# A dynamic convolution and a two-layer MLP: the leftover 64 rows of the first layer as two matmuls on halves of the array, chunks taken in groups of four

## The chip, the cores and the metric

The kernel runs on one core of a Trainium2 chip. The metric is the device time of one execution in microseconds (us); less is better. The profile and the trace come from one further execution, recorded by the hardware profiler.

## The reference

`x` is 4 x 4096 tokens of 192 features, `weight_gen` gives 8 heads x 7 taps for each token, and the MLP has weights of 192 x 2048 and 2048 x 192, all fp32. Cut to what matters:

```python
w = exp(weight_gen - max(weight_gen)); w = w / (sum(w) + 1e-09)      # over the 7 taps
out[b, s, h] = sum_k w[b, s, h, k] * x_pad[b, s + k, h]              # 8 heads of 24 features
h = out.reshape(16384, 192) @ w_in                                   # 2048 hidden features
return maximum(0.01 * h, h) @ w_out
```

## The kernel before, in words

**Precision.** Each fp32 operand of a matmul is scaled by a power of two and split into two fp16 numbers, a high part and a low part (the rest). A product is then the sum of high x high, high x low and low x high.

**Tiles.** The 16384 tokens make 32 tiles (`TILES`) of 512 (`NT`: 4 tokens in each of 128 partitions). The 2048 hidden features make 16 chunks of 128 (`NF`); `f` counts the chunks of a tile, `m` the tiles.

**TensorE** (PE, lines 591 to 706). For each chunk, `hidden` (L605) makes the first layer in five matmuls of 512 columns into one of two PSUM banks `h_ps`. The 192 input features are more than the 128 rows of the array. The first 128 take `whA` and `wlA` against the high part of x (L608, L609) and `whA` against its low part (L612). The other 64 are laid out so that high and low parts of x alternate in the 128 rows, and meet `whD` (L610) and `wlD` (L611), whose rows hold each of the 64 weight rows twice. `project` (L635) makes the second layer, for each of the four groups `j` of 128 tokens: one matmul of 384 columns with the high part `gh` as stationary operand against both parts of `w_out` (L626), and one of 192 columns with `gl` against the high part (L631). The sums lie in four banks of `out_ps`, the products with the high and with the low part of `w_out` side by side. The first layer runs three chunks ahead (`LAG`) of the second. In slot 11 of 16 come twelve transposes of the next tile's x (L599, L602).

**ScalarE** (ACT, L274). For each chunk, `leaky` reads `h_ps` twice: `gh` in fp16 (L304) and `g` in fp32 (L306). Once a tile it makes the high part of x (L295), copies the transposed x out of PSUM (L300), and in `copy_out` (L309) moves the half of `out_ps` that holds the products with the low part of `w_out` to `stage` (L317). Every second tile it takes the exponentials of the taps (L284).

**VectorE** (DVE, L368) makes the convolution of the coming tiles (`convolve`, L420: products L433, sums L440, then scales), the softmax of the taps, the low part of x (L464), one in four of the low parts `gl = g - gh` (L473), and in `sum_out` (L476) adds the two halves of the output (L480). **GpSimd** (POOL, L215) makes the other three of four `gl` (L227). Rings of four chunks hold `gh`, `gl` and `g`.

**Order.** Everything is placed by hand in 16 slots a tile: `CONV_IN_SLOT`, `SOFTMAX_IN_SLOT`, `X_HI_SLOT`, `X_LO_SLOT`, `TRANSPOSE_SLOT`. In tile 0 the weights are split in pieces as well, each of four chunks: the high part by ScalarE (L279, `HI_IN_SLOT`), then the low part by VectorE (L459, `LO_IN_SLOT`); TensorE waits for the pieces in `step` (L661). The **SP** queue (L235) loads x and taps a chunk of two tiles at a time, and stores each tile (`store`, L259).

## Time and profile before

| what | value |
|---|---|
| median of 3 runs | 1132.56 us (1132.48 to 1132.85) |
| profiled execution: its time | 1132.38 us |
| its span, first to last instruction | 1130.6 us |
| mean granted TensorE clock | 0.994 of full speed |
| busy: PE, PE weight loads, DVE, ACT, POOL | 96%, 57%, 74%, 61%, 51% of the span |
| moved by DMA | 43.02 MB, 38 GB/s on the mean |

How to read it: the span leaves out what lies around the instructions (1132.38 - 1130.6 = 1.8 us). Busy shares are means over the whole span, and matmuls overlap each other in the pipeline, so the distance from the start of one to the start of the next (the pitch) tells what one costs, not its own duration.

### The profile page before, as it was taken

How to read it: one execution, taken by the hardware profiler on the slowest of the kernel's cores; microseconds unless marked ns; L12 is line 12 of the kernel's file. 1: busy time of each engine (PE TensorE's matmuls, PEld its weight loads, DVE VectorE, ACT ScalarE, POOL GpSimd, SP SyncE). 2: the span in 40 equal slices, each digit the busy share in tenths (PEclk: the TensorE clock that was granted, in tenths of full speed). 3: DMA queues.
4: the chain of work that ended last, by engine and by line, in shares of the span. 5: the costliest groups of instructions: out<-in, count | busy, mean ns of one | idle time of the engine just before them, and what ended most of it. 6: DMA issues, size and time to landing. Idle time of an engine off the chain costs nothing.

```text
span 1130.6 us, 17224 instructions
## 1 busy us (share of the span) xinstructions
PE 1091.0 (96%) x7064; PEld 646.3 (57%) x7064; DVE 837.8 (74%) x1126; ACT 694.5 (61%) x1348; POOL 574.8 (51%) x392
## 2 busy tenths in 40 slices
PE   2689999999999999999999999999999999999998
PEld 0346565665555565556556555656555556556564
DVE  7877877768687677877768787777878767787730
ACT  3556666656666666656666666666666666666664
POOL 0245555555555545455555555555555555555533
PEclk9889999999999999999999999999999999999999
DMA  7010010101001010100101001010200101000000
GB/s 243 1 58 14 18 70 15 71 1 72 14 15 72 15 58 15 53 34 15 72 5 67 15 15 72 14 72 1 72 14 15 72 14 58 15 15 15 15 15 14
DMA packets 12102, 43.02 MB, mean 38 GB/s; under 512 B 1276, under 2 KB 5372, under 8 KB 9848
## 3 DMA queue, kind: packets, MB, share of 16 engines
q1 hardware_dynamic: 11900, 41.64, 10.0%
q8 instruction: 55, 0.90, 0.4%
q10 hardware_dynamic: 124, 0.29, 0.2%
q14 instruction: 23, 0.19, 0.1%
HBM read 29.34 MB, written 12.58 MB: 37 GB/s over the span
## 4 chain that ended last, share of the span: by engine, by line
PE 93%; DVE 5%; ACT 1%; DMA 0%; issue 0%; ACTq 0%; POOL 0%; DVEq 0%; POOLq 0%
PE out_ps L626 29%; PE out_ps L631 15%; PE h_ps L608 10%; PE h_ps L609 10%; PE h_ps L610 10%; PE h_ps L612 10%; PE h_ps L611 10%; PE t_ps L599 1%; DVE conv L440 1%; DVE prod L433 1%; PE t_ps L602 1%; DMA xbuf<-in_x_dram 0%; DVE wo L459 0%; ACT xs L295 0%; DVE xs L464 0%; DVE conv L433 0%
## 5 line engine op out<-in xcount | busy, mean ns | idle before, releaser
L227 POOL TENSOR_TENSOR gl<-g,gh 128x512 f16<-128x512 f32 x384 | 572.8, 1495 | 548.7 <-ACT g L306 548.6
L304 ACT ACTIVATE gh<-h_ps 128x512 f16<-128x512 f32 x512 | 304.9, 596 | 389.2 <-PE h_ps L612 385.2
L626 PE MATMUL out_ps<-wo,gh 128*128 128x384 f16 x2048 | 423.4, 327 | 0.0
L306 ACT ACTIVATE g<-h_ps 128x512 f32<-128x512 f32 x512 | 302.9, 592 | 0.0
L626 PEld LDWEIGHTS out_ps<-wo,gh 128*128 128x128 f16 x2048 | 198.7, 98 | 168.7 <-issue 1.9
L433 DVE TENSOR_TENSOR prod<-xbuf,taps 128x768 f32<-128x768 f32 x192 | 274.1, 1440 | 0.0
L631 PE MATMUL out_ps<-wo,gl 128*128 128x192 f16 x2048 | 258.6, 246 | 0.6 <-DVE gl L473 0.6
L473 DVE TENSOR_TENSOR gl<-g,gh 128x512 f16<-128x512 f32 x128 | 105.2, 822 | 180.4 <-ACT g L306 180.4
L631 PEld LDWEIGHTS out_ps<-wo,gl 128*128 128x128 f16 x2048 | 186.1, 98 | 71.7 <-DVE gl L473 1.0
L440 DVE TENSOR_TENSOR conv<-conv,prod 128x768 f32<-128x768 f32 x192 | 209.2, 1089 | 0.6
L608 PE MATMUL h_ps<-xT,whA 128*128 128x512 f16 x512 | 194.8, 380 | 7.3 <-DVE wo L459 3.8
L612 PE MATMUL h_ps<-xT,whA 128*128 128x512 f16 x512 | 194.8, 380 | 0.0
L609 PE MATMUL h_ps<-xT,wlA 128*128 128x512 f16 x512 | 194.8, 380 | 0.0
L610 PE MATMUL h_ps<-xT,whD 128*128 128x512 f16 x512 | 194.8, 380 | 0.0
L611 PE MATMUL h_ps<-xT,wlD 128*128 128x512 f16 x512 | 194.8, 380 | 0.0
L611 PEld LDWEIGHTS h_ps<-xT,wlD 128*128 128x128 f16 x512 | 50.3, 98 | 60.9 <-issue 0.8
L610 PEld LDWEIGHTS h_ps<-xT,whD 128*128 128x128 f16 x512 | 50.3, 98 | 60.9 <-issue 0.8
L612 PEld LDWEIGHTS h_ps<-xT,whA 128*128 128x128 f16 x512 | 50.2, 98 | 60.9 <-issue 0.8
L480 DVE SCALAR_TENSOR_TENSOR stage<-out_ps,out_scale,stage 128x192 f32<-128x192 f32 x128 | 44.6, 411 | 52.2 <-ACT stage L317 52.2
L608 PEld LDWEIGHTS h_ps<-xT,whA 128*128 128x128 f16 x512 | 50.2, 98 | 12.7 <-DVE wo L459 4.0
L317 ACT ACTIVATE stage<-out_ps,out_scale 128x192 f32<-128x192 f32 x128 | 43.4, 422 | 16.8 <-PE out_ps L631 16.8
L609 PEld LDWEIGHTS h_ps<-xT,wlA 128*128 128x128 f16 x512 | 50.2, 98 | 4.2 <-issue 0.3
(54 smaller groups left out, 428.3 us busy)
## 6 DMA issues: line engine op xcount, KB each, us to landing
xbuf<-in_x_dram SPq DMA_DIRECT2D x15, 1344.0 KB, 5.6
out_dram<-stage SPq DMA_DIRECT2D x32, 384.0 KB, 2.3
taps<-in_weight_gen_dram SPq DMA_DIRECT2D x16, 224.0 KB, 5.8
rawO<-in_moe_w_out_dram SPq DMA_DIRECT2D x4, 384.0 KB, 9.9
rawA<-in_moe_w_in_dram SPq DMA_DIRECT2D x1, 1024.0 KB, 7.5
rawD<-in_moe_w_in_dram SPq DMA_DIRECT2D x2, 512.0 KB, 8.7
xbuf<-in_x_dram SPq DMA_DIRECT2D x2, 384.0 KB, 5.7
xbuf<-in_x_dram SPq DMA_DIRECT2D x2, 72.0 KB, 4.2
```

Source lines behind the costliest of these rows:

```text
L227: nc.gpsimd.tensor_tensor(gl[:, f % G_RING, :], g[:, f % G_RING, :], gh[:, f % G_RING, :], ALU.subtract).then_inc(s_gl_p, 1)
L304: nc.scalar.activation(gh[:, f % G_RING, :], h_ps[f % 2][:], ACT.Prelu, scale=SHRINK, alpha=SLOPE).then_inc(s_gh, 1)
L306: nc.scalar.activation(g[:, f % G_RING, :], h_ps[f % 2][:], ACT.Prelu, scale=SHRINK, alpha=SLOPE).then_inc(s_g, 1)
L433: ins = nc.vector.tensor_tensor(dst.rearrange("p (r g) -> p r g", g=G), rows, w.to_broadcast([P, SUB * H, G]), ALU.mult)
L440: ins = nc.vector.tensor_tensor(acc, acc, prod[:, k % PRODS, :], ALU.add)
L608: nc.tensor.matmul(dst, whA[:, c], xT[:, par, 0, :], start=True, stop=False)
L609: nc.tensor.matmul(dst, wlA[:, c], xT[:, par, 0, :], start=False, stop=False)
L610: nc.tensor.matmul(dst, whD[:, c], xT[:, par, 1, :], start=False, stop=False)
L611: nc.tensor.matmul(dst, wlD[:, c], xT[:, par, 1, :], start=False, stop=False)
L612: nc.tensor.matmul(dst, whA[:, c], xT[:, par, 2, :], start=False, stop=True).then_inc(s_h, 1)
L626: nc.tensor.matmul(out_ps[:, j, 0:2 * D], gh[:, f % G_RING, j * P:(j + 1) * P], wo[:, f, :, :], start=f == 0, stop=False)
L631: ins = nc.tensor.matmul(out_ps[:, j, 0:D], gl[:, f % G_RING, j * P:(j + 1) * P], wo[:, f, 0, :], start=False, stop=f == NF - 1)
```

## The change

**First layer.** In place of five matmuls of 512 columns over 128 rows, a chunk has four of those and one of 512 columns over 64 rows. x is transposed in three blocks: its first 128 features (high), then features 128 to 191 (high) with features 0 to 63 (low), then features 64 to 191 (low). `whA` and `wlA` meet the first block, `whX` the second, `whC` the third. What is left, the low part of the last 64 weight rows against the high part of the last 64 features of x, is a matmul over 64 rows. For an even chunk it takes rows 0 to 63 of the array, for an odd chunk rows 64 to 127, from copies of `wlX` and of the transposed x (`xT_again`) that DMAs put there. The product of the two low parts of these 64 features, which `wlD` brought with it, is not made any more.

**Groups.** `hidden` and `project` work on groups of four chunks: sixteen full matmuls into four banks `h_ps`, then the four 64-row ones; then the second layer of the group before. The first layer is one group ahead. The rings hold eight chunks.

**Second layer.** The products with both parts of `w_out` are summed in the same 192 columns: two matmuls of 192 columns in place of one of 384. `out_ps` has two banks, each with the sums of two groups of tokens. `sum_out` is gone: ScalarE copies the finished sums to `stage`.

**Order.** Slots are replaced by four steps a tile; 9 of the 18 operations of a convolution run a tile ahead (5 before). VectorE makes `gl` of the last chunk of each group. The SP queue has `move_weights` (three DMAs for each of four pieces) and `move_x` (one DMA a tile), and a store is issued one tile later in its program.

The diff, cut to its core (lines that rename `whD`, `rawD` and the rings are left out):

```diff
-LAG = 3
-G_RING = 4
+GROUP = 4
+RING = 2 * GROUP
 PRODS = 3
 SLOPE = 0.01
-LO_PERIOD = 4
...
+CONV_AHEAD_IN = {2: 4, 3: 5}
+CONV_AHEAD = sum(CONV_AHEAD_IN.values())
+CONV_IN = {0: 4, 1: N_CONV - CONV_AHEAD - 4}
 
 N_SOFTMAX = 6
-SOFTMAX_IN_SLOT = {2: (0,), 3: (1,), 6: (2, 3), 7: (4,), 8: (5,)}
-EXP_SLOT = 4
+SOFTMAX_IN = {0: (0, 1), 1: (2, 3, 4, 5)}
...
+        xT_again = sb("xT_again", [P, 2, NT], F16)
...
-        gh = sb("gh", [P, G_RING, NT], F16)
-        gl = sb("gl", [P, G_RING, NT], F16)
-        g = sb("g", [P, G_RING, NT])
-
-        h_ps = [ps(f"h_ps{b}", [P, NT]) for b in range(2)]
+        gh = sb("gh", [P, RING, NT], F16)
+        gl = sb("gl", [P, RING, NT], F16)
+        g = sb("g", [P, RING, NT])
+
+        h_ps = [ps(f"h_ps{b}", [P, NT]) for b in range(GROUP)]
         t_ps = ps("t_ps", [P, 2, NT], F16)
         t2_ps = ps("t2_ps", [P, 2, NT], F16)
-        out_ps = ps("out_ps", [P, SUB, 512])
+        out_ps = ps("out_ps", [P, 2, 512])
...
+        HI_IN = [3, 3, 1, 0]
...
+        LO_IN = [3, 3, 1, 0]
...
+            return f % GROUP == GROUP - 1
+
+        def out_of(j):
+            return out_ps[:, j // 2, j % 2 * D:(j % 2 + 1) * D]
...
-            for half in range(2):
-
-                sp.dma_start(rawD[half:P:2, :], w_in[P:D, :]).then_inc(s_rawD, DMA)
+
+            sp.dma_start(rawX[0:DR, :], w_in[P:D, :]).then_inc(s_rawX, DMA)
+            sp.dma_start(rawX[DR:P, :], w_in[0:DR, :]).then_inc(s_rawX, DMA)
...
+            def move_weights(n):
+
+                c = slice(n * PIECE, (n + 1) * PIECE)
+                sp.wait_ge(s_w_hi, hi_done(("X", n)))
+                sp.dma_start(whC[0:DR, c], whA[DR:P, c]).then_inc(s_w_moved[n], DMA)
+                sp.dma_start(whC[DR:P, c], whX[0:DR, c]).then_inc(s_w_moved[n], DMA)
+                sp.wait_ge(s_w_lo, LO_ORDER.index(("X", n)) + 1)
+                sp.dma_start(wlX[DR:P, c], wlX[0:DR, c]).then_inc(s_w_moved[n], DMA)
+
+            def move_x(t):
+
+                sp.wait_ge(s_xT_a, t + 1)
+                sp.dma_start(xT_again[DR:P, t % 2, :], xT[0:DR, t % 2, 1, :]).then_inc(s_xT_again, DMA)
...
+            move_weights(0)
+            move_x(0)
+            for n in range(1, N_PIECES):
+                move_weights(n)
             for m in range(TILES):
+                if m > 0:
+                    store(m - 1)
                 if m % 2 == 0 and m // 2 + 2 < CHUNKS:
 
                     c = m // 2
                     sp.wait_ge(s_conv, (c * 2 + 2) * N_CONV)
                     load_chunk(c + 2, c % 2)
-                store(m)
+                if m + 1 < TILES:
+                    move_x(m + 1)
+            store(TILES - 1)
...
+            def leaky(n):
+
+                for f in range(n % NG * GROUP, (n % NG + 1) * GROUP):
+                    act.wait_ge(s_h, n // NG * NF + f + 1)
+                    nc.scalar.activation(gh[:, f % RING, :], h_ps[f % GROUP][:], ACT.Prelu, scale=SHRINK, alpha=SLOPE
+                                         ).then_inc(s_gh, 1)
+                    nc.scalar.activation(g[:, f % RING, :], h_ps[f % GROUP][:], ACT.Prelu, scale=SHRINK, alpha=SLOPE
+                                         ).then_inc(s_g, 1)
...
-                    nc.scalar.activation(stage[:, u, j, :], out_ps[:, j, D:2 * D], ACT.Copy,
-                                         scale=out_scale[:, u, j:j + 1]).then_inc(s_out_part, 1)
-
-            def step(m):
+                    nc.scalar.activation(stage[:, u, j, :], out_of(j), ACT.Copy, scale=out_scale[:, u, j:j + 1]
+                                         ).then_inc(s_out_free, 1)
+
+            def step(n):
+
+                m, i = n // NG, n % NG
                 last = m == TILES - 1
...
+                if i == 0 and m > 0:
+                    copy_out(m - 1)
+                if i == 0 and m % 2 == 0 and m + 2 < TILES:
+                    exp_taps(m // 2 + 1)
+                if i == 1 and not last:
+                    hi_of_x(m + 1)
+                if m == 0:
+                    for piece in HI_ORDER[HI_FIRST + sum(HI_IN[:i]):HI_FIRST + sum(HI_IN[:i + 1])]:
+                        split_hi(piece)
+                if i == 2 and not last:
+                    take_transposed(m + 1)
+                if n + 1 < NG * TILES:
+                    leaky(n + 1)
...
+                        if t >= 2:
+
+                            dve.wait_ge(s_out_free, SUB * (t - 1))
...
-                    nc.vector.scalar_tensor_tensor(xs[:, j, :, 1], conv[:, j, :], x_scale[:, j:j + 1], xs[:, j, :, 0],
+                    nc.vector.scalar_tensor_tensor(xs[:, j, D:2 * D], conv[:, j, :], x_scale[:, j:j + 1], xs[:, j, 0:D],
...
-            def sum_out(m):
-                u = m % 2
-                for j in range(SUB):
-                    dve.wait_ge(s_out_part, SUB * m + j + 1)
-                    nc.vector.scalar_tensor_tensor(stage[:, u, j, :], out_ps[:, j, 0:D],
-                                                   out_scale[:, u, j:j + 1], stage[:, u, j, :],
-                                                   ALU.mult, ALU.add).then_inc(s_out_free, 1)
...
+                if m % 2 == 0 and m + 2 < TILES:
+                    c = m // 2 + 1
+                    for k in SOFTMAX_IN.get(i, ())[0:2]:
+                        if k == 0:
+
+                            dve.wait_ge(s_chunk[c % 2], DMA * (c + 1))
+                        softmax(c, k)
+                if i in CONV_IN and not last:
+                    for k in range(CONV_IN[i]):
+                        convolve(m + 1, CONV_AHEAD + sum(CONV_IN[b] for b in range(i)) + k)
+                if i in CONV_AHEAD_IN and m + 2 < TILES:
+                    if i == 2 and m % 2 == 0:
+
+                        dve.wait_ge(s_softmax, N_SOFTMAX * (m // 2 + 1))
+                    for k in range(CONV_AHEAD_IN[i]):
+                        if k == 1:
+                            lo_of_g(n * GROUP + GROUP - 1, n % NG * GROUP + GROUP - 1)
+                        convolve(m + 2, sum(CONV_AHEAD_IN[b] for b in range(2, i)) + k)
+                else:
+                    lo_of_g(n * GROUP + GROUP - 1, n % NG * GROUP + GROUP - 1)
+                if m % 2 == 0 and m + 2 < TILES:
+                    for k in SOFTMAX_IN.get(i, ())[2:]:
+                        softmax(m // 2 + 1, k)
+                if m == 0:
+                    for piece in LO_ORDER[LO_FIRST + sum(LO_IN[:i]):LO_FIRST + sum(LO_IN[:i + 1])]:
+                        split_lo(piece)
+                if i == 1 and not last:
+                    lo_of_x(m + 1)
+                if i == 2 and not last:
+                    take_transposed(m + 1)
...
+            def hidden(n):
+                m, i = n // NG, n % NG
+                par = m % 2
+                fs = range(i * GROUP, (i + 1) * GROUP)
+                if i == 0:
+                    pe.wait_ge(s_xT_a, m + 1)
+                    pe.wait_ge(s_xT_v, m + 1)
+                for f in fs:
+                    c = slice(f * P, (f + 1) * P)
+                    dst = h_ps[f % GROUP][:]
+                    if n > 0:
+
+                        pe.wait_ge(s_g, m * NF + f - GROUP + 1)
+                    nc.tensor.matmul(dst, whA[:, c], xT[:, par, 0, :], start=True, stop=False)
+                    nc.tensor.matmul(dst, wlA[:, c], xT[:, par, 0, :], start=False, stop=False)
+                    nc.tensor.matmul(dst, whX[:, c], xT[:, par, 1, :], start=False, stop=False)
+                    nc.tensor.matmul(dst, whC[:, c], xT[:, par, 2, :], start=False, stop=False)
+
+                if i == 0:
+                    pe.wait_ge(s_xT_again, DMA * (m + 1))
+                for f in fs:
+                    c = slice(f * P, (f + 1) * P)
+                    if f % 2 == 0:
+                        ins = nc.tensor.matmul(h_ps[f % GROUP][:], wlX[0:DR, c], xT[0:DR, par, 1, :],
+                                               start=False, stop=True)
+                    else:
+                        ins = nc.tensor.matmul(h_ps[f % GROUP][:], wlX[DR:P, c], xT_again[DR:P, par, :],
+                                               start=False, stop=True)
+                    ins.then_inc(s_h, 1)
...
+                    pe.wait_ge(s_gl_v, (m * NF + f) // GROUP + 1)
...
+                    pe.wait_ge(s_gl_p, (m * NF + f) // GROUP * (GROUP - 1) + f % GROUP + 1)
...
+            def project(n):
+                m, i = n // NG, n % NG
+                fs = range(i * GROUP, (i + 1) * GROUP)
+                for f in fs:
+                    pe.wait_ge(s_gh, m * NF + f + 1)
+                    for j in range(SUB):
+                        if f == 0 and m > 0 and j % 2 == 0:
+
+                            pe.wait_ge(s_out_free, SUB * (m - 1) + j + 2)
+                        for part in range(2):
+                            nc.tensor.matmul(out_of(j), gh[:, f % RING, j * P:(j + 1) * P], wo[:, f, part, :],
+                                             start=f == 0 and j % 2 == 0 and part == 0, stop=False,
+                                             skip_group_check=True)
+                for f in fs:
                     wait_lo(m, f)
-                    project_lo(f, range(SUB))
-                elif f == NF - 1:
-                    project_hi(f, (0, 1))
-                    wait_lo(m, f)
-                    project_lo(f, (0, 1)).then_inc(s_out_ps, 1)
-                    project_hi(f, (2, 3))
-                    project_lo(f, (2, 3)).then_inc(s_out_ps, 1)
-                else:
-                    project_hi(f, range(SUB))
-                    wait_lo(m, f)
-                    project_lo(f, range(SUB))
+                    for j in range(SUB):
+                        ins = nc.tensor.matmul(out_of(j), gl[:, f % RING, j * P:(j + 1) * P], wo[:, f, 0, :],
+                                               start=False, stop=f == NF - 1, skip_group_check=True)
+                        if f == NF - 1 and j % 2 == 1:
+                            ins.then_inc(s_out_ps, 1)
...
+            def wait_w_in(n):
+
+                wait_piece(("A", n))
+                wait_piece(("X", n))
+                pe.wait_ge(s_w_moved[n], 3 * DMA)
+
+            def step(n):
+                m, i = n // NG, n % NG
+                if n + 1 < NG:
+                    wait_w_in(n + 1)
+                if n + 1 < NG * TILES:
+                    hidden(n + 1)
+                if i == 2 and m + 1 < TILES:
+                    transpose_tile(m + 1)
+                if n < NG:
+                    wait_piece(("O", n))
+                project(n)
```

## Rows read from the trace of the kernel before

**Rows 1.** The page: busy time of the engines, and the chain that ended last

```profile
PE 1091.0 (96%) x7064; PEld 646.3 (57%) x7064; DVE 837.8 (74%) x1126; ACT 694.5 (61%) x1348; POOL 574.8 (51%) x392
...
PE 93%; DVE 5%; ACT 1%; DMA 0%; issue 0%; ACTq 0%; POOL 0%; DVEq 0%; POOLq 0%
```

**Rows 2.** The windows: stretch, us, busy us (count) by engine, PE clock, DMA, GB/s

```profile
40.00:80.00 40.00, 31.48 (x171) 17.16 (x170) 35.15 (x46) 21.18 (x39) 16.03 (x11) 0.85 0.11 41
80.00:500.00 420.00, 420.00 (x2746) 250.25 (x2745) 319.63 (x422) 264.19 (x518) 223.90 (x150) 1.00 0.10 36
```

**Rows 3.** The timeline of PE, one chunk: start us, us, engine, line

```profile
501.26 0.38 PE L608 MATMUL h_ps<-xT,whA 128*128 128x512 f16 x1
501.48 0.38 PE L609 MATMUL h_ps<-xT,wlA 128*128 128x512 f16 x1
501.69 0.38 PE L610 MATMUL h_ps<-xT,whD 128*128 128x512 f16 x1
501.91 0.38 PE L611 MATMUL h_ps<-xT,wlD 128*128 128x512 f16 x1
502.13 0.38 PE L612 MATMUL h_ps<-xT,whA 128*128 128x512 f16 x1
502.34 0.81 PE L626 MATMUL out_ps<-wo,gh 128*128 128x384 f16 x4
502.99 0.49 PE L631 MATMUL out_ps<-wo,gl 128*128 128x192 f16 x4
503.32 0.38 PE L608 MATMUL h_ps<-xT,whA 128*128 128x512 f16 x1
```

**Rows 4.** The page's costliest groups: xcount, busy us, mean ns, idle before, its releaser

```profile
L227 POOL TENSOR_TENSOR gl<-g,gh 128x512 f16<-128x512 f32 x384 | 572.8, 1495 | 548.7 <-ACT g L306 548.6
L304 ACT ACTIVATE gh<-h_ps 128x512 f16<-128x512 f32 x512 | 304.9, 596 | 389.2 <-PE h_ps L612 385.2
...
L306 ACT ACTIVATE g<-h_ps 128x512 f32<-128x512 f32 x512 | 302.9, 592 | 0.0
...
L433 DVE TENSOR_TENSOR prod<-xbuf,taps 128x768 f32<-128x768 f32 x192 | 274.1, 1440 | 0.0
...
L473 DVE TENSOR_TENSOR gl<-g,gh 128x512 f16<-128x512 f32 x128 | 105.2, 822 | 180.4 <-ACT g L306 180.4
L631 PEld LDWEIGHTS out_ps<-wo,gl 128*128 128x128 f16 x2048 | 186.1, 98 | 71.7 <-DVE gl L473 1.0
L440 DVE TENSOR_TENSOR conv<-conv,prod 128x768 f32<-128x768 f32 x192 | 209.2, 1089 | 0.6
...
L480 DVE SCALAR_TENSOR_TENSOR stage<-out_ps,out_scale,stage 128x192 f32<-128x192 f32 x128 | 44.6, 411 | 52.2 <-ACT stage L317 52.2
...
L317 ACT ACTIVATE stage<-out_ps,out_scale 128x192 f32<-128x192 f32 x128 | 43.4, 422 | 16.8 <-PE out_ps L631 16.8
```

**Rows 5.** The timeline of PE in the start

```profile
29.67 0.61 PE L599 MATMUL t_ps<-ident,xs 128*128 128x128 f16 x8
30.11 0.39 PE L602 MATMUL t_ps<-ident,xs 128*128 128x128 f16 x4
...
32.63 0.38 PE L608 MATMUL h_ps<-xT,whA 128*128 128x512 f16 x1
...
37.71 0.39 PE L608 MATMUL h_ps<-xT,whA 128*128 128x512 f16 x1 [2.76 <-ACT g L306]
...
38.74 0.63 PE L612 MATMUL h_ps<-xT,whA 128*128 128x512 f16 x1
39.16 0.63 PE L608 MATMUL h_ps<-xT,whA 128*128 128x512 f16 x1
...
53.47 0.61 PE L608 MATMUL h_ps<-xT,whA 128*128 128x512 f16 x1 [3.81 <-DVE wo L459]
```

**Rows 6.** The timeline of VectorE in the start

```profile
40.68 1.63 DVE L459 SCALAR_TENSOR_TENSOR wlD<-rawD,w_scale,whD 128x512 f16<-128x512 f32 x1
...
42.84 1.91 DVE L433 TENSOR_TENSOR conv<-xbuf,taps 128x768 f32<-128x768 f32 x1
...
47.28 0.95 DVE L433 TENSOR_TENSOR prod<-xbuf,taps 128x768 f32<-128x768 f32 x1
48.15 1.91 DVE L440 TENSOR_TENSOR conv<-conv,prod 128x768 f32<-128x768 f32 x1
```

**Rows 7.** The page's DMA issues: KB each, us from issue to landing

```profile
out_dram<-stage SPq DMA_DIRECT2D x32, 384.0 KB, 2.3
```

**Rows 8.** The timeline at the end, all engines

```profile
1125.57 1.36 ACT L317 ACTIVATE stage<-out_ps,out_scale 128x192 f32<-128x192 f32 x4 [2.43 <-PE out_ps L631]
1125.61 0.33 PE L631 MATMUL out_ps<-wo,gl 128*128 128x192 f16 x2
```

More of the change, by code:

```diff
@@ L66, in dynconv_mlp @@
     DR = D - P
-    assert DR == P // 2 and NF == 16 and sum(CONV_IN_SLOT) == N_CONV and K == 7
+    NG = NF // GROUP
+    assert DR == P // 2 and NF == 16 and sum(CONV_IN.values()) + CONV_AHEAD == N_CONV and K == 7
     assert TILES % 2 == 0 and PART_SEQ == 32
@@ L88, in dynconv_mlp @@
         wlA = sb("wlA", [P, FF], F16)
-        whD = sb("whD", [P, FF], F16)
-        wlD = sb("wlD", [P, FF], F16)
+        whX = sb("whX", [P, FF], F16)
+        whC = sb("whC", [P, FF], F16)
+        wlX = sb("wlX", [P, FF], F16)
         wo = sb("wo", [P, NF, 2, D], F16)
@@ L142, in dynconv_mlp @@
         s_w_lo = sem("s_w_lo")
+        s_w_moved = [sem(f"s_w_moved{n}") for n in range(4)]
         s_softmax0 = sem("s_softmax0")
@@ L171, in dynconv_mlp @@
             c = slice(n * PIECE, (n + 1) * PIECE)
-            pieces["D", n] = (rawD[:, c], whD[:, c], wlD[:, c])
+            pieces["X", n] = (rawX[:, c], whX[:, c], wlX[:, c])
         for n in range(N_PIECES):
@@ L362, in _ @@
                 split_hi(piece)
-            for f in range(LAG):
-                leaky(f, f)
-            for m in range(TILES):
-                step(m)
+            leaky(0)
+            for n in range(NG * TILES):
+                step(n)
+            copy_out(TILES - 1)
         @block.vector
@@ L457, in split_lo @@
                 raw, hi, lo = pieces[piece]
+                rows = slice(0, DR) if piece[0] == "X" else slice(0, P)
+                n = 1 if piece[0] == "O" else 0
                 dve.wait_ge(s_w_hi, hi_done(piece))
-                nc.vector.scalar_tensor_tensor(lo, raw, scale_of(piece), hi, ALU.mult, ALU.subtract).then_inc(s_w_lo, 1)
+                nc.vector.scalar_tensor_tensor(lo[rows], raw[rows], w_scale[rows, n:n + 1], hi[rows], ALU.mult,
+                                               ALU.subtract).then_inc(s_w_lo, 1)
             def lo_of_x(t):
@@ L584, in _ @@
             dve.wait_ge(s_chunk[0], DMA)
-            lo_of_g(0, 0)
             for n in range(CONV_AHEAD):
                 convolve(1, n)
-            for m in range(TILES):
-                step(m)
+            for n in range(NG * TILES):
+                step(n)
         @block.tensor
@@ L618, in wait_lo @@
             def wait_lo(m, f):
                 if lo_on_vector(f):
-                    pe.wait_ge(s_gl_v, m * LO_V[-1] + LO_V[f])
+                    pe.wait_ge(s_gl_v, (m * NF + f) // GROUP + 1)
                 else:
-                    pe.wait_ge(s_gl_p, m * LO_P[-1] + LO_P[f])
-            def project_hi(f, subs):
-                for j in subs:
-                    nc.tensor.matmul(out_ps[:, j, 0:2 * D], gh[:, f % G_RING, j * P:(j + 1) * P], wo[:, f, :, :],
-                                     start=f == 0, stop=False)
@@ L697, in _ @@
             warm_up(WARM_UP[1])
-            wait_piece(("A", 0))
-            wait_piece(("D", 0))
-            operands(0)
-            for f in range(LAG):
-                if f >= 2:
-                    pe.wait_ge(s_g, f - 1)
-                hidden(f, f, 0)
-            for m in range(TILES):
-                step(m)
+            wait_w_in(0)
+            hidden(0)
+            for n in range(NG * TILES):
+                step(n)
 _INS = ["x", "weight_gen", "moe_w_in", "moe_w_out"]
```

149 lines of the change are left out of this document (19 added, 130 removed).

## The prediction

> **What bounds the kernel now.** First the page: TensorE is busy for 96% of the span, and 93% of the chain that ended last runs through it [rows 1]. Then the windows: from 80 to 500 us it has no idle time, at full clock [rows 2]. So in the steady part only TensorE's own work counts, and the other engines matter when they come too late for it. Then the timeline of one chunk, read by pitch [rows 3]: five matmuls of 512 columns start 0.216 us apart (1.08 us), four of 384 take 0.65, four of 192 take 0.33; one chunk 2.06 us. Twelve transposes start 0.055 us apart [rows 5], 0.67 us a tile. A tile is 16 x 2.06 + 0.67 = 33.6 us. The windows agree: 2746 matmuls in 420 us at 220 a tile are 33.65 us a tile [rows 2]. All 512 chunks and 31 sets of transposes make 1055 + 21 = 1076 us.
>
> The rest of the span is start and end. The first layer begins at 32.6 us [rows 5] and 4.8 us lie behind the last matmuls [rows 8], so 1130.6 - 32.6 - 4.8 - 1076 = 17 us are lost in the start, in waits for weight pieces and in stretches at half clock that follow them (pitch 0.42 us in place of 0.216) [rows 5]. The mean clock from 40 to 80 us is 0.85 [rows 2].
>
> **The change part by part.** *First layer.* A chunk has four full matmuls, 4 x 0.216 = 0.864 us. Its fifth uses half of the rows. If two such run at once, a pair costs one pitch, 0.108 us a chunk. The saving is 0.108 us x 512 = 55.3 us, all of it on the path.
>
> *Second layer.* Eight matmuls of 192 columns take the place of four of 384: 8 x 0.0825 = 0.66 us against 0.65. This holds although each brings its own weight load, because the 192-column matmuls of before do so too, at the same pitch [rows 3], and the transposes load every 0.055 us [rows 5]. Cost 0.01 us x 512 = 5.1 us. Steady balance: 1.962 us a chunk against 2.06, -50.2 us.
>
> *Going in and out of halves.* Each of the 128 groups goes from matmuls over 128 rows to ones over 64, and back: 256 changes of shape. The trace of before has none: every matmul in it uses all rows. This is the term that decides. Lower end: nothing, as the array takes these matmuls like any others (a gain is excluded; no work is saved by it beyond what is counted). Upper end: the earlier matmul must leave the pipeline (a 512-column one lasts 0.380 us and hands over after 0.216, so its tail is 0.164 us [rows 3]), and only then is the next stationary operand loaded (0.098 us [rows 4]): 0.262 us. Between them stands one of the two alone. I take 0.098 us, an uncovered weight load: of the rows at hand it is the one nearest to the middle of the interval, and it is work that certainly has to be done in the other shape. 256 x 0.098 = 25.1 us.
>
> The trace shows, for matmuls of one shape, that a load is hidden behind the matmul before it: load and matmul keep the pitch of the columns [rows 3]. The Trainium skill speaks against this change here: by "TensorEngine Tiling (Array Packing)", Key Properties, going from one tiling mode to another drains the TensorE. No row here shows that. By the rule the term would be that of the tail, with or without the load behind it; both are rivals below.
>
> *ScalarE, VectorE and GpSimd in the steady part.* Group time on TensorE: first layer 16 x 0.216 + 2 x 0.216 = 3.89 us, second 48 x 0.0825 = 3.96 us, together 7.85 us. ScalarE works off four banks in 4 x (0.596 + 0.592) = 4.75 us [rows 4], the first bank 1.2 us after the group's first layer ends. That bank is wanted back after 3.96 us and the fourth after 3.96 + 3 x 0.864 = 6.6 us: hidden. The copies of the output (4 x 0.422 us) begin at 4.75 us and give back the second bank of sums at 6.5 us, before it is wanted at 7.85: hidden. The transposed x lets ScalarE begin 1.7 us later in one group of four; its fourth bank is then free at 6.4 + 0.7 us behind, against 7.3: hidden, but with little room. GpSimd has three subtractions of 1.5 us a group [rows 4], done by about 5.8 us, needed after 7.85 + 2.6: hidden. The sums by VectorE, 44.6 us [rows 4], go; they were not on the path.
>
> *The new DMAs.* One of 64 KB a tile copies the transposed x. A store of six times its size lands in 2.3 us [rows 7], so it is there 2.6 us after ScalarE's copy; the 64-row matmuls that want it come some 6 us after that copy: hidden. On the SP queue it stands behind a store and a chunk load whose conditions were met a whole group earlier, and behind the wait for ScalarE's copy nothing is queued that is wanted soon.
>
> *Start.* The first group begins at 32.6 us as before and ends at 36.5. The second waits for the low parts of the second pieces, ready at about 41.5 us [rows 6], and then for the new copy of `wlX`, another 2.3 us: 43.9 us. TensorE has been idle for 7 us, so I count this group at half clock for most of its length, 6.4 us, to 50.2. The second layer of group 0 wants the `gl` that VectorE makes; in front of it stand 9 + 4 convolution operations at 0.87 us [rows 6], more beside GpSimd, and two of the softmax: about 57 us. The third pieces (high parts by ScalarE behind the taps' exponentials, low parts by VectorE, then the copy) come at 61.5 us, after another idle stretch: 6.5 us of first layer, 4 of second, so the fourth group's first layer begins at 72 us. Done by then are 3 x 3.89 + 2 x 3.96 = 19.6 us of work; lost 72 - 32.6 - 19.6 = 19.8 us, against 17: +2 us, uncertain by 5.
>
> *End.* The four copies are no longer half done when TensorE stops: +0.3 us; the sums behind them go.
>
> Sum: 1130.6 - 50.2 + 2 + 0.3 = 1082.7 us of span without the changes of shape, 1107.8 with them, plus 1.8 outside it: **1110 us**. The profiled execution (1132.38) stands 0.2 below the median, less than I can resolve. Break-even is 48 / 256 = 0.187 us a change.
>
> **The rivals.** *Free changes of shape*: 1084.5 us. For it: the matmuls are like any others for the queue. *A full tail a change, the load hidden in it*: 256 x 0.164 = 42 us, 1126.5 us. *Tail and load*: 67 us, 1151.6 us, slower; it decides from 0.187 us on. This is the price at which nothing of one shape overlaps with the other. Against it: today's loads run beside matmuls throughout [rows 3]. These two are what the Trainium skill's rule on modes, named above, would give. *The halves do not run at once*: +0.216 us x 2 a group, 55.3 us: 1140 us without any other price. No row shows two matmuls at once; those of odd and even chunks write different banks and read different partitions, so nothing that they share in memory stands against it. By the Trainium skill ("TensorE: Matmul & The Clock Gate", Part 3) matmuls on different row tiles start some 4 ns apart, which no row here shows. *VectorE comes too late with the fourth `gl`*: between those of two groups at a tile's edge stand eight convolution operations (five sums, three products: 9.8 us), on even tiles two of the softmax (1.2), and its own 0.8: 11.8 us. Beginning at 4.75 us behind the first layer of the one group it ends at 16.6, wanted at 2 x 7.85 + 3.6 = 19.3. Were all eight at 1.91 us, as beside GpSimd, in place of 0.95 without it [rows 6], it would be 3 us late, in 16 tiles, 45 us: about 1155. The means [rows 4] already hold the usual share of it.
>
> **How the numbers follow.** Uncovered load, 1110 us: 0.34. Free: 0.20. Tail: 0.20. Tail and load: 0.16. Halves one after the other: 0.05. VectorE late: 0.05. Faster by over 0.2% (2.3 us, about what a measurement of this kernel can tell from no change) takes the first two, nearly all of the third and parts of the gaps between: 0.72. Slower 0.24, within 0.2% 0.04. The range goes from just below the free case, 1082, to 1146 us; outside are the full price and VectorE late.
>
> **What would show it.** In the trace after: eight 192-column matmuls at 0.0825 us (else the second layer's term is off); two 64-row matmuls starting together and the next pair 0.216 us later (else the halves rival); the gap from the last full matmul to the first half, and from the last half to the first of the second layer, over the pitch, which prices the change directly: 0, 0.1, 0.16 or 0.26. TensorE idle before its `gl` matmuls, released by VectorE, shows the last rival; the fourth group's first layer at 72 us shows the start. I am wrong if the two gaps together are above 0.37 us a group.

## The result, and the profile after

| | before | after |
|---|---|---|
| median of the runs | 1132.7 us (4 runs, 1132.48 to 1134.86) | 1112.8 us (4 runs, 1112.15 to 1113.25) |
| ratio, 95% interval | | 0.982 (0.9803 to 0.9837) |
| span of the profiled execution | 1130.6 us | 1111.1 us |
| mean granted TensorE clock | 0.994 | 0.992 |

The change makes the kernel 20 us faster, 1.8%. The prediction said 1110 us, 1082 to 1146.

The page of the changed kernel, to be read against [rows 1, 4]: engines, the chain that ended last, and the costliest groups (xcount, busy us, mean ns, idle before).

```profile
PE 1066.3 (96%) x9112; PEld 736.9 (66%) x9112; DVE 788.0 (71%) x998; ACT 659.9 (59%) x1348; POOL 492.0 (44%) x392
...
PE 94%; DVE 3%; DMA 1%; ACT 1%; SPq 0%; issue 0%; POOL 0%; ACTq 0%; POOLq 0%
...
L227 POOL TENSOR_TENSOR gl<-g,gh 128x512 f16<-128x512 f32 x384 | 490.0, 1304 | 610.6 <-ACT g L330 610.6
L328 ACT ACTIVATE gh<-h_ps 128x512 f16<-128x512 f32 x512 | 319.1, 623 | 232.3 <-PE h_ps L646 232.3
L666 PE MATMUL out_ps<-wo,gh 128*128 128x192 f16 x4096 | 359.8, 246 | 0.0
```

TensorE is still the chain. It has 2048 matmuls more and 25 us less busy time. The other engines have idle time before nearly every burst of work, but it costs nothing while TensorE does not wait.

The timeline of TensorE around the 64-row matmuls of one group, with the weight loads (PEld), against [rows 3]:

```profile
505.94 0.38 PE L636 MATMUL h_ps<-xT,whC 128*128 128x512 f16 x1
506.25 0.09 PEld L643 LDWEIGHTS h_ps<-xT,wlX 64*128 64x128 f16 x1 [0.42 <-issue]
506.25 0.09 PEld L646 LDWEIGHTS h_ps<-xT_again,wlX 64*128 64x128 f16 x1
506.25 0.39 PE L643 MATMUL h_ps<-xT,wlX 64*128 64x512 f16 x1
506.25 0.39 PE L646 MATMUL h_ps<-xT_again,wlX 64*128 64x512 f16 x1
...
506.48 0.38 PE L643 MATMUL h_ps<-xT,wlX 64*128 64x512 f16 x1
506.48 0.38 PE L646 MATMUL h_ps<-xT_again,wlX 64*128 64x512 f16 x1
506.78 0.45 PEld L614 LDWEIGHTS t_ps<-ident,xs 128*128 128x128 f16 x8 [0.42 <-issue]
506.79 0.62 PE L614 MATMUL t_ps<-ident,xs 128*128 128x128 f16 x8
```

Four things are to be seen. The two matmuls on the halves start together (0.003 us apart on the mean); that they also run at once, e2 shows by its time. The next pair starts 0.23 us later, one pitch and about 0.01 (0.226 us on the mean over 110 groups of this trace). The way into the halves takes 0.31 us from start to start, and the way out 0.31 as well, 0.095 over the pitch of 0.216 each. And the load for the first half does not stand one matmul ahead, as loads within one shape do, but at the same time as its own matmul, with 0.42 us of idle time of the loader before it. The last full matmul ends its own pitch at 505.94 + 0.216 us and the next full shape begins at 506.79, so the block of halves takes 0.63 us a group.

The windows, against [rows 2]:

```profile
80.00:500.00 420.00, 420.00 (x3628) 292.52 (x3626) 309.34 (x383) 258.21 (x534) 192.76 (x154) 1.00 0.11 38
```

A tile now has 16 x 17 + 12 = 284 matmuls, so 3628 of them in 420 us are 32.88 us a tile, against 33.65 before: 0.77 us x 32 = 25 us less in the steady part, in which TensorE is never idle. The spans differ by 19.5, so start and end gave back 5 us.

The start of the changed kernel, TensorE's timeline, against [rows 5]:

```profile
34.35 0.38 PE L633 MATMUL h_ps<-xT,whA 128*128 128x512 f16 x1
...
45.33 0.57 PE L633 MATMUL h_ps<-xT,whA 128*128 128x512 f16 x1 [5.13 <-DMA wlX<-wlX]
...
58.64 0.50 PE L672 MATMUL out_ps<-wo,gl 128*128 128x192 f16 x4 [3.74 <-DVE gl L502]
64.79 0.58 PE L633 MATMUL h_ps<-xT,whA 128*128 128x512 f16 x1 [5.65 <-DMA wlX<-wlX]
...
75.05 0.38 PE L633 MATMUL h_ps<-xT,whA 128*128 128x512 f16 x1
```

The three waits are those that the prediction worked out: twice for the copied `wlX`, once for the `gl` behind the convolutions. The fourth group begins at 75.05 us; 72 was predicted.

### The profile page after: what moved, and what is told of

It is laid out like the page before. It is cut to its first block, busy times and chain, and to the rows that moved or that the text cites. A ratio compares the mean times of both kernels' runs of the same rounds, so it can differ in the third digit from the quotient of the medians.

```text
span 1111.1 us, 21269 instructions
## 1 busy us (share of the span) xinstructions
PE 1066.3 (96%) x9112; PEld 736.9 (66%) x9112; DVE 788.0 (71%) x998; ACT 659.9 (59%) x1348; POOL 492.0 (44%) x392
## 4 chain that ended last, share of the span: by engine, by line
PE 94%; DVE 3%; DMA 1%; ACT 1%; SPq 0%; issue 0%; POOL 0%; ACTq 0%; POOLq 0%
PE out_ps L666 31%; PE out_ps L672 15%; PE h_ps L633 10%; PE h_ps L634 10%; PE h_ps L635 10%; PE h_ps L636 10%; PE h_ps L643 6%; PE t_ps L614 2%; DMA rawX<-in_moe_w_in_dram 1%; DVE conv L463 1%; PE t_ps L617 1%; DVE prod L456 1%; DVE wo L487 0%; DVE w_abs L547 0%; DVE wlX L487 0%
## 5 line engine op out<-in xcount | busy, mean ns | idle before, releaser
L227 POOL TENSOR_TENSOR gl<-g,gh 128x512 f16<-128x512 f32 x384 | 490.0, 1304 | 610.6 <-ACT g L330 610.6
L666 PE MATMUL out_ps<-wo,gh 128*128 128x192 f16 x4096 | 359.8, 246 | 0.0
L666 PEld LDWEIGHTS out_ps<-wo,gh 128*128 128x128 f16 x4096 | 332.7, 98 | 40.7 <-issue 40.7
L456 DVE TENSOR_TENSOR prod<-xbuf,taps 128x768 f32<-128x768 f32 x192 | 208.0, 1096 | 0.0
L633 PE MATMUL h_ps<-xT,whA 128*128 128x512 f16 x512 | 195.8, 382 | 10.8 <-DMA wlX<-wlX 10.8
L635 PE MATMUL h_ps<-xT,whX 128*128 128x512 f16 x512 | 195.7, 382 | 0.0
L636 PE MATMUL h_ps<-xT,whC 128*128 128x512 f16 x512 | 195.6, 382 | 0.0
L672 PE MATMUL out_ps<-wo,gl 128*128 128x192 f16 x2048 | 190.1, 246 | 3.7 <-DVE gl L502 3.7
L643 PE MATMUL h_ps<-xT,wlX 64*128 64x512 f16 x256 | 77.0, 381 | 0.0
L646 PE MATMUL h_ps<-xT_again,wlX 64*128 64x512 f16 x256 | 77.0, 381 | 0.0
## 6 DMA issues: line engine op xcount, KB each, us to landing
rawX<-in_moe_w_in_dram SPq DMA_DIRECT2D x2, 512.0 KB, 11.1
```

What stands on the lines that cost most here:

```text
L227: nc.gpsimd.tensor_tensor(gl[:, f % RING, :], g[:, f % RING, :], gh[:, f % RING, :], ALU.subtract).then_inc(s_gl_p, 1)
L456: ins = nc.vector.tensor_tensor(dst.rearrange("p (r g) -> p r g", g=G), rows, w.to_broadcast([P, SUB * H, G]), ALU.mult)
L633: nc.tensor.matmul(dst, whA[:, c], xT[:, par, 0, :], start=True, stop=False)
L635: nc.tensor.matmul(dst, whX[:, c], xT[:, par, 1, :], start=False, stop=False)
L636: nc.tensor.matmul(dst, whC[:, c], xT[:, par, 2, :], start=False, stop=False)
L643: ins = nc.tensor.matmul(h_ps[f % GROUP][:], wlX[0:DR, c], xT[0:DR, par, 1, :], start=False, stop=True)
```

## The experiments

The theory: a change of shape costs 0.095 us over the pitch, 256 times; pairs run at once; TensorE carries it all. Rivals: the changes of shape are free and the gain leaks elsewhere (groups, second layer, start); the price is the weight load itself. There are four sets of runs (the change itself; e1 to e4; e5 to e7; e8), and each has the kernel before beside it on the same chip. Its median was 1132.7 to 1135.2 us in the four sets, so a difference between two sets is good to some 2.5 us.

### e1_full_fifth: the halves undone

```diff
-                    if f % 2 == 0:
-                        ins = nc.tensor.matmul(h_ps[f % GROUP][:], wlX[0:DR, c], xT[0:DR, par, 1, :],
-                                               start=False, stop=True)
-                    else:
-                        ins = nc.tensor.matmul(h_ps[f % GROUP][:], wlX[DR:P, c], xT_again[DR:P, par, :],
-                                               start=False, stop=True)
-                    ins.then_inc(s_h, 1)
+                    nc.tensor.matmul(h_ps[f % GROUP][:], wlX[:, c], xT[:, par, 1, :],
+                                     start=False, stop=True).then_inc(s_h, 1)
...
-                sp.dma_start(wlX[DR:P, c], wlX[0:DR, c]).then_inc(s_w_moved[n], DMA)
+                sp.wait_ge(s_zeros, 1)
+                sp.dma_start(wlX[DR:P, c], zeros[0:DR, :]).then_inc(s_w_moved[n], DMA)
```

> The changed kernel (1112.8 us) with the halves undone: in the same place of each group stand four matmuls of 512 columns over all 128 rows (the copy of wlX in rows 64 to 127 is zeros, so the sums are the same). Price of a change of shape, read from the trace after: the four 64-row matmuls with their two changes take 0.31 + 0.23 + 0.31 - 0.216 = 0.63 us a group; four full ones take 4 x 0.216 = 0.86. This theory expects +0.23 x 128 = 29 us: 1142 us. Rival: the changes of shape are free and what is missing of the gain is lost in the groups and the second layer. Then undoing the halves costs the whole 55 us: 1168 us.

Measured: 1140.6 us (6 runs, 1139.5 to 1141.3), 1.0055 of before (1.0038 to 1.0071), +28 us on the changed kernel. That is the 29 us of the theory; the rival's 55 are excluded. Its trace has, in the place of the halves:

```profile
501.67 0.38 PE L640 MATMUL h_ps<-xT,whC 128*128 128x512 f16 x1
501.88 1.03 PE L646 MATMUL h_ps<-xT,wlX 128*128 128x512 f16 x4
502.75 2.80 PE L665 MATMUL out_ps<-wo,gh 128*128 128x192 f16 x32
```

The way in is one pitch here (0.21 us) and the four take 0.87 us, four pitches: in the same order of work, without a change of shape, there is no gap. Without the halves the rewritten kernel is slower than before: groups, second layer and start together bring nothing by themselves.

### e2_halves_serial: all on one half

```diff
-                    if f % 2 == 0:
-                        ins = nc.tensor.matmul(h_ps[f % GROUP][:], wlX[0:DR, c], xT[0:DR, par, 1, :],
-                                               start=False, stop=True)
-                    else:
-                        ins = nc.tensor.matmul(h_ps[f % GROUP][:], wlX[DR:P, c], xT_again[DR:P, par, :],
-                                               start=False, stop=True)
-                    ins.then_inc(s_h, 1)
+                    nc.tensor.matmul(h_ps[f % GROUP][:], wlX[0:DR, c], xT[0:DR, par, 1, :],
+                                     start=False, stop=True).then_inc(s_h, 1)
```

> The changed kernel with all four 64-row matmuls of a group on rows 0 to 63, so that none can run beside another. If the pairs really run at once, this costs two more matmuls of 512 columns a group, less 0.015 us for the second pair's later start: (1.054 - 0.634) x 128 = 54 us, 1167 us. If pairs share a record but not the array, nothing changes: 1113 us. The gaps into and out of the 64-row shape should stay 0.095 us over the pitch if they belong to the shape, and go if they come from the switch between two halves.

Measured: 1166.65 us (4 runs, 1166.5 to 1167.0), +54 us. Its timeline of TensorE in one group, where the four 64-row matmuls stand as one row:

```profile
511.10 0.38 PE L636 MATMUL h_ps<-xT,whC 128*128 128x512 f16 x1
511.42 1.03 PE L642 MATMUL h_ps<-xT,wlX 64*128 64x512 f16 x4
512.38 1.82 PE L661 MATMUL out_ps<-wo,gh 128*128 128x192 f16 x20
```

The way in still takes 0.32 us, and from the first of the four to the next shape are 0.96 us, 4 x 0.216 + 0.095. So the pairs really overlap in the array, and the gaps belong to the change of shape, not to the second half.

### e3_pairs: twice as many changes of shape

```diff
-                for f in fs:
+                for pair in (fs[:2], fs[2:]):
+                    for f in pair:
...
-                if i == 0:
-                    pe.wait_ge(s_xT_again, DMA * (m + 1))
-                for f in fs:
+                    if i == 0:
+                        pe.wait_ge(s_xT_again, DMA * (m + 1))
+                    for f in pair:
```

> The changed kernel with the 64-row matmuls in two batches of two, each behind its two chunks: four changes of shape a group in place of two, all else as it was. Price of each change 0.095 us: a group takes 2 x (0.31 + 0.31 - 0.216) = 0.81 us for them in place of 0.63, +22 us, 1135 us. Changes free, or the price hidden beside other work: 1113 us. A full tail and load for each (0.262 us): +67 us less what is in the 0.63 already, 1150 us or more.

Measured: 1139.8 us (6 runs, 1138.9 to 1140.1), +27 us. The timeline of one of its batches:

```profile
506.32 0.38 PE L637 MATMUL h_ps<-xT,whC 128*128 128x512 f16 x1
506.63 0.39 PE L643 MATMUL h_ps<-xT,wlX 64*128 64x512 f16 x1
506.63 0.39 PE L646 MATMUL h_ps<-xT_again,wlX 64*128 64x512 f16 x1
506.95 0.39 PE L634 MATMUL h_ps<-xT,whA 128*128 128x512 f16 x1
507.18 0.38 PE L635 MATMUL h_ps<-xT,wlA 128*128 128x512 f16 x1
```

In 0.31, out 0.32, and the second matmul in the new shape another 0.01 us late (0.23 from start to start): 0.43 us a batch over the last full matmul's own pitch, 0.86 a group. Counted alike, with that hundredth behind the way out, the changed kernel has 0.64, and 0.22 x 128 = 28 us. My 22 left out the hundredth after each change and the one on the way out. The price is paid per change, and with batches of two the kernel is slower than the one before (1.0048, 1.0033 to 1.0063) and within 1 us of the one with four full matmuls (e1).

### e4_no_halves: the 64-row matmuls left out

```diff
-                    nc.tensor.matmul(dst, whC[:, c], xT[:, par, 2, :], start=False, stop=False)
-
+                    nc.tensor.matmul(dst, whC[:, c], xT[:, par, 2, :], start=False, stop=True).then_inc(s_h, 1)
                 if i == 0:
                     pe.wait_ge(s_xT_again, DMA * (m + 1))
-                for f in fs:
...
```

> The changed kernel without the 64-row matmuls: the product of the low part of the last 64 weight rows with the high part of x is left out. If TensorE bounds and the block of halves costs 0.63 us a group on the path: -81 us, 1032 us. Rival: another engine is close behind (ScalarE's 4.75 us a group and its copies, or VectorE's gl), and takes over as the bound: less than -60 us, with TensorE idle before matmuls on h_ps or gl.

Measured: 1062.5 us (4 runs, 1062.3 to 1062.6), -50 us and not -81. One of TensorE's waits in it (us in total, times, longest), and one of these times in its timeline:

```profile
PE out_ps L662 <- DVE gl L502: 27.0, 31, 1.3
...
628.56 1.15 PE L662 MATMUL out_ps<-wo,gl 128*128 128x192 f16 x12
630.68 0.50 PE L662 MATMUL out_ps<-wo,gl 128*128 128x192 f16 x4 [0.97 <-DVE gl L502]
```

Each group is 0.63 us shorter, as expected, but once a tile TensorE now waits about 0.9 us for the fourth `gl`, 27 us in all. -81 + 27 is -54. The rest is in how idle time is counted: it begins at the modelled end of a matmul's record, 0.16 us behind its pitch (0.246 - 0.0825). Twelve pitches from 628.56 end at 629.55 us and the next matmul starts at 630.68, so 1.13 us are lost where the row says 0.97. 31 x 0.16 us are 5 us more, which gives -49. The rival holds here: VectorE stands close behind TensorE. In the changed kernel this wait came once, in the start; the steady part has none. So the block of halves costs its 0.63 us a group, and of what leaving it out would give, VectorE keeps about two fifths (32 of 81 us).

### e5_split_second: the second layer's split alone, in the kernel before

```diff
-                    nc.tensor.matmul(out_ps[:, j, 0:2 * D], gh[:, f % G_RING, j * P:(j + 1) * P], wo[:, f, :, :],
-                                     start=f == 0, stop=False)
+                    for part in range(2):
+                        nc.tensor.matmul(out_ps[:, j, part * D:(part + 1) * D], gh[:, f % G_RING, j * P:(j + 1) * P],
+                                         wo[:, f, part, :], start=f == 0 and part == 0, stop=False,
+                                         skip_group_check=True)
```

> The kernel before with one part of the change alone: each matmul of 384 columns of the second layer as two of 192, into the same two column ranges. By the pitches 0.65 to 0.66 us a chunk: +5 us (2048 more matmuls at 0.0025 us each), 1138 us. Rival: the additional weight loads show (ten more of 0.098 us hidden with less room): a chunk of 0.7 us or more for these eight, over +20 us.

Measured: 1138.7 us (5 runs, 1137.8 to 1139.5), 1.0045 of before (1.0031 to 1.006), +5.4 us. The timeline of one chunk:

```profile
506.46 0.82 PE L627 MATMUL out_ps<-wo,gh 128*128 128x192 f16 x8
507.12 0.49 PE L633 MATMUL out_ps<-wo,gl 128*128 128x192 f16 x4
```

Eight matmuls take 0.66 us, with eight loads in place of four (the expectation says "ten more"; they are four more a chunk), all hidden.

### e6_narrow_load: is it the load?

```diff
-                    nc.tensor.matmul(dst, whC[:, c], xT[:, par, 2, :], start=False, stop=False)
+                    nc.tensor.matmul(dst, whC[:, c], xT[:, par, 2, :], start=False, stop=True)
...
-                        ins = nc.tensor.matmul(h_ps[f % GROUP][:], wlX[0:DR, c], xT[0:DR, par, 1, :],
-                                               start=False, stop=True)
+                        ins = nc.tensor.matmul(h_ps[f % GROUP][0:96, :], wlX[0:DR, f * P:f * P + 96],
+                                               xT[0:DR, par, 1, :], start=False, stop=True, skip_group_check=True)
...
-                        ins = nc.tensor.matmul(h_ps[f % GROUP][:], wlX[DR:P, c], xT_again[DR:P, par, :],
-                                               start=False, stop=True)
+                        ins = nc.tensor.matmul(h_ps[f % GROUP][0:96, :], wlX[DR:P, f * P:f * P + 96],
+                                               xT_again[DR:P, par, :], start=False, stop=True, skip_group_check=True)
```

> The changed kernel with stationary operands of 96 columns in place of 128 in the 64-row matmuls; a quarter of their product is left out. It tells what the 0.095 us at a change of shape is. If it is the load, not hidden there, the gap moves with the length of the load's record, whichever way that goes for 96 columns. If it is a wait before the load for the matmul ahead, the gap stays 0.31 us whatever the load takes. Both expect the time within 10 us of 1113.

Measured: 1116.9 us (2 runs). Its timeline, loads included:

```profile
507.78 0.38 PE L636 MATMUL h_ps<-xT,whC 128*128 128x512 f16 x1
508.09 0.12 PEld L643 LDWEIGHTS h_ps<-xT,wlX 64*96 64x96 f16 x1 [0.42 <-issue]
508.09 0.41 PE L643 MATMUL h_ps<-xT,wlX 64*96 64x512 f16 x1
...
508.35 0.38 PE L643 MATMUL h_ps<-xT,wlX 64*96 64x512 f16 x1
...
508.66 0.62 PE L614 MATMUL t_ps<-ident,xs 128*128 128x128 f16 x8
```

A stationary operand of 96 columns loads more slowly (record 0.12 us against 0.09), and the way in stays 0.31 us; the load's own record starts only then, so what stands before it is not the load. The longer load shows behind the first matmul instead: 0.26 us to the next pair against 0.23. 0.03 us x 128 is 3.8 us. The kernel is 4 us slower, but with two executions and a difference of up to 2.5 us between sets the time alone would not show that; the trace does. So there are two terms: a wait of 0.095 us that stands before the load and does not depend on it, and behind it the part of the load that no matmul covers, some 0.01 us for 128 columns and 0.04 for 96. For the way out, where the load is the same in both kernels, this was not tested.

### e7_start_first and e8_start_second: another order in tile 0

The schedule of tile 0, in the changed kernel. For VectorE (the other two engines alike: ScalarE makes the high parts right behind `leaky(0)` and `leaky(1)`, TensorE does the second layer of groups 2 and 3 before the transposes of tile 1):

```diff
-            split_lo(LO_ORDER[2])
+            for piece in LO_ORDER[2:4]:
+                split_lo(piece)
...
-            for n in range(CONV_AHEAD):
-                convolve(1, n)
-            for n in range(NG * TILES):
-                step(n)
+            first(0, 1, 2)
+            lo_of_g(GROUP - 1, GROUP - 1)
+            for piece in LO_ORDER[5:8]:
+                split_lo(piece)
+            first(3, 4, 5, 6)
+            lo_of_g(2 * GROUP - 1, 2 * GROUP - 1)
+            first(7, 8)
+            for piece in LO_ORDER[8:12]:
+                split_lo(piece)
...
+            for n in range(NG, NG * TILES):
+                step(n)
```

Here `first(...)` is `convolve(1, n)` for each n, and both orders of pieces become A, X, O for each n with A and X ahead.

> The changed kernel with another order in tile 0 only: the weight pieces are split before the convolutions of tile 1, gl before them too, the pieces A and X ahead of O, and the second layer of groups 2 and 3 ahead of the transposes. If the start's loss (fourth group's first layer at 75.05 us) is VectorE's and ScalarE's order in the start, as I worked out, the first four groups run nearly without waits, and the first layer of tile 1 begins near 71 us with one more group of the second layer done: -14 us, 1099 us. Rival: the start is bound by VectorE's whole work up to the low part of x for tile 1, which no order shortens: less than -5 us.

Measured: 1114.4 us (5 runs, 1109.4 to 1114.95): nothing gained on the median, and the number is the rival's. Three of the five took 1114.4 us or more at a mean clock of 0.992 (the changed kernel: 1112.2 to 1113.3 at 0.992 and 0.993), two 1109.4 and 1109.8 at 0.997. The trace of a run of 1114.4 us shows where the gain went, first TensorE's waits, then GpSimd's timeline:

```profile
PE out_ps L710 <- DVE gl L513: 5.3, 1, 5.3
PE out_ps L710 <- POOL gl L227: 4.8, 1, 4.8
```

```profile
41.12 5.27 POOL L227 TENSOR_TENSOR gl<-g,gh 128x512 f16<-128x512 f32 x3 [38.30 <-ACT g L330]
47.06 21.44 POOL L227 TENSOR_TENSOR gl<-g,gh 128x512 f16<-128x512 f32 x6 [0.67 <-ACT g L330]
```

Six subtractions took GpSimd 21.4 us, where six take under 8 on the mean. From 46.9 to 69 us VectorE had no idle time in this run. The fourth group's first layer began at 64.9 us in place of 75.05, and the waits for the weight pieces went (one of 1.65 us was left of two of over 5), but two waits for `gl` came in their place, the second at 99 us. A second version is meant to meet both:

```diff
             lo_of_g(2 * GROUP - 1, 2 * GROUP - 1)
+            dve.wait_ge(s_gl_p, 2 * (GROUP - 1))
...
-            for n in range(CONV_AHEAD):
+            for n in range(5):
+                convolve(2, n)
+            lo_of_g(5 * GROUP - 1, GROUP - 1)
+            for n in range(5, CONV_AHEAD + CONV_IN[0]):
                 convolve(2, n)
-            for n in range(NG, NG * TILES):
+            for n in range(NG + 1, NG * TILES):
```

> The run with the reordered start, with its two late waits met: in it TensorE waited 4.8 us for GpSimd's gl, which had taken 21.4 us for six subtractions beside an unbroken row of VectorE work, and 5.3 us for the gl that VectorE made behind nine convolution operations of tile 2. Here VectorE pauses until GpSimd has made the gl of group 1, and makes its own gl of group 4 behind five of these operations. If the two engines' turns decide, both waits go and the start gains what it lost: 1104 to 1107 us. Rival: the work of VectorE up to tile 2 is the bound and only moves: 1112 us or more, with a wait for gl elsewhere before 130 us.

Measured: 1108.8 us (5 runs, 1104.3 to 1109.2), 0.9775 of before (0.976 to 0.979), against 0.982 (0.9803 to 0.9837) for the change as it was. The version beats both kernels: 4 us better than the change, a little short of what was hoped. The profiled execution is the fastest of the five, 1104.3 us. In it both waits for `gl` are gone. Of what TensorE still waits for, two rows, and then GpSimd's timeline:

```profile
PE h_ps L675 <- DMA wlX<-wlX: 6.2, 3, 2.9
PE h_ps L675 <- ACT g L330: 2.1, 2, 1.1
```

```profile
46.38 9.22 POOL L227 TENSOR_TENSOR gl<-g,gh 128x512 f16<-128x512 f32 x3 [2.48 <-ACT g L330]
57.47 14.36 POOL L227 TENSOR_TENSOR gl<-g,gh 128x512 f16<-128x512 f32 x6 [1.87 <-ACT g L330]
```

The fourth group's first layer began at 61.4 us, so the order of VectorE's work was a part of the start's loss. What the new wait of VectorE did is not shown: GpSimd had made the three `gl` of group 1 at 55.60 us, before VectorE came to that wait behind its own `gl` (54.51 + 1.63 us), and VectorE has no idle time there. Up to that point the two versions have the same order, and the same three subtractions took 9.2 us here and some 16.5 in e7 (TensorE got the third at 63.67 us). So in this execution the first of the two waits went without the edit that was meant for it. Of the other four no trace was kept.

Nor is it shown that all of the 4 us are the order's. The mean clock was 0.995 in those four and 0.992 to 0.993 in the changed kernel; 0.003 of 1110 us is 3.3 us at full clock, an estimate of the most that this can make. Whether the tighter start brings the better clock with it, these runs do not tell. The copies of `wlX` by DMA cost 6.2 us even so (1.7 in e7); a second load of these 64 rows straight into rows 64 to 127 was not tried.

## Why the prediction was right

*First layer, 55.3 us.* Right: pairs start together (trace), and e2 prices their overlap at 54 us.

*Second layer, 5.1 us.* Right: e5 measured 5.4.

*Changes of shape, 25.1 us.* The size was right (2 x 0.095 + 0.01 us a group, 26 us), and the reason was not. I took it for an uncovered weight load, because the row of 0.098 us lay nearest to the middle of the interval. It did not: the middle of 0 to 0.262 is 0.131, and 0.098 and 0.164 lie equally far from it, as they must, since their sum is the upper end. With the tail in its place the forecast would have been 1126.5 us. e6 shows a wait that stands before the load and stays when the load gets longer; of the load itself only some 0.01 us shows. That the numbers 0.095 and 0.098 are alike is chance, and so the time of 1110 us was hit by luck in the term that decides; the sign and the range did not need it, as the price stayed under the 0.187 us of break-even. The rule of the Trainium skill that I set against it ("TensorEngine Tiling (Array Packing)", Key Properties: a change of tiling mode drains the TensorE) is in kind what the trace shows: the loader idle for 0.42 us, and nothing of the new shape pulled ahead. In size it was too dear as I read it, as a full tail of 0.164 us; the first half starts 0.31 us behind a matmul whose record lasts 0.38. Whether the 0.095 us are the array's part of the pipeline running empty, I did not measure.

*Steady part in sum.* Predicted 16 x 1.962 + 0.67 + 8 x 0.098 = 32.85 us a tile, measured 32.88.

*Other engines.* Hidden, as said. The rival of the late fourth `gl` was not far: 0.63 us less a group and it appears (e4), although on the trace VectorE is busy for only 71%. My slack of 2.7 us at a tile's edge was too large: two groups shorter by 0.63 us each were enough to lose 1.0 us there.

*Start, +2 us.* The term that was off: the fourth group's first layer began at 75.05 us and not at 72. What it waits for at the end is VectorE's work, which has no idle time from 38.45 us until the third `wlX` is done and its copy is issued:

```profile
41.50 1.64 DVE L487 SCALAR_TENSOR_TENSOR wlX<-rawX,w_scale,whX 64x512 f16<-64x512 f32 x1
...
56.94 1.64 DVE L502 TENSOR_TENSOR gl<-g,gh 128x512 f16<-128x512 f32 x1
58.50 1.90 DVE L487 SCALAR_TENSOR_TENSOR wo<-rawO,w_scale,wo 128x768 f16<-128x768 f32 x1
60.33 1.63 DVE L487 SCALAR_TENSOR_TENSOR wlA<-rawA,w_scale,whA 128x512 f16<-128x512 f32 x1
61.89 0.73 DVE L487 SCALAR_TENSOR_TENSOR wlX<-rawX,w_scale,whX 64x512 f16<-64x512 f32 x1
...
62.65 0.46 SPq L266 DMA_DIRECT2D wlX<-wlX  x1
```

The second `wlX` was done at 43.1 us and not at 41.5. VectorE came to it 0.8 us later than to the like operation before (41.50 against 40.68), and I had counted that operation some 0.8 us too short, though it takes 1.63 us in [rows 6] as well. From there to VectorE's `gl` of group 0 all went as counted (58.6 us against 57). Then the third pieces and their copy took 6.2 us in place of my 4.5: two of the three splits took 1.90 and 1.63 us, where the like ones at 67 and 68 us took 1.02 and 0.75, and beside them GpSimd made three subtractions (56.16 to 61.42 us). From the third group to the fourth it is 10.3 us, as counted.

The first group began 1.7 us late (34.35 against 32.6 us), where the loads of `rawX` landed later (11.1 us against 8.7 for `rawD`, by the pages' DMA issues; ScalarE waited 2.5 us for it in place of 0.6), and it ran for 3.3 us at half clock, which I had not counted. On TensorE neither lengthened anything: it waited 5.1 us behind that group. The page's row:

```profile
rawX<-in_moe_w_in_dram SPq DMA_DIRECT2D x2, 512.0 KB, 11.1
```

These 3 us are nearly all of the 3.3 us between the span of 1107.8 that the sum gave and the 1111.1 of the trace.

## What to carry to other kernels

Two matmuls over 64 rows do run at once on the array's halves, but each change between 64 and 128 rows costs about 0.1 us of TensorE, so gather as many 64-row matmuls between two changes as PSUM banks allow: in fours they paid here, in twos not. Splitting a matmul of 384 columns in two of 192 cost 0.0025 us each. When a part of a schedule is made tighter, read the waits anew: here the engine next behind the bound kept two fifths of the gain (e4), and beside a gapless row of VectorE work GpSimd became so slow that TensorE waited for it (e7).

## What the runs showed that I had not expected

GpSimd's subtraction, 1.3 us on the mean in the changed kernel, took 3.6 us each beside an unbroken row of VectorE operations (e7, six in 21.4 us). The changed kernel has such a stretch too; where VectorE is idle (71.9 to 75.0 us), three take 3.4 us:

```profile
41.18 12.30 POOL L227 TENSOR_TENSOR gl<-g,gh 128x512 f16<-128x512 f32 x3 [38.37 <-ACT g L330]
...
72.12 3.39 POOL L227 TENSOR_TENSOR gl<-g,gh 128x512 f16<-128x512 f32 x3 [10.71 <-ACT g L330]
```

That the two engines hold each other up is read from such pairs of rows; no run here changes it alone, and how long the three take varies with the same order of work (9.2 us in e8, some 16.5 in e7).

The granted clock in the first 80 us differs from run to run. The profiled execution of e8 never left the upper level (mean clock 1.0, 1104.3 us), its four others had a mean clock of 0.995 and took 1108.6 to 1109.2 us. In the changed kernel's trace the level of 1.2 GHz was granted from 35.0 to 38.3 us (0.52 on the mean of that stretch), though TensorE had been running since 24.4 us with one gap of 2.3 us just before. A start that is some us shorter can so be hidden by the clock: the executions of e7, one and the same kernel, lie up to 5.6 us apart by it.
